# Moving the low parts of the first expert's weights from VectorE to GpSimd

## The chip, the cores and the metric

The program runs on one core of a Trainium2 chip. The metric is the device time of one execution in microseconds (us). Before the change three runs took 922.83, 923.97 and 923.83 us, median 923.83 us.

## The reference

Three layers follow each other, all in fp32: attention, a feed-forward layer and a mixture of experts.

```python
x = (out_up + out_local)            # attention, 4 x 8 heads, 576 x 64; x becomes (2304, 512)
h = x @ w_in                        # (512, 2048)
g = h * tanh(softplus(h))
x = g @ w_out                       # (2048, 512)
logits = x @ w_gate + modality_bias[modality_id]      # 8 experts
e_idx = argmax(logits, axis=1)
out[token] = gate_w * (relu(x @ w1[e]) @ w2[e])       # w1[e] (512, 1024), w2[e] (1024, 512)
```

## The kernel before

Products in fp32 are made of three products each: every operand is split into a high part, rounded to the matmul's format, and a low part, the rest (raw minus high). ScalarE copies the high part (a cast), another engine subtracts to get the low part, and TensorE adds up high x high, high x low and low x high.

The feed-forward layer works on 6 blocks of 384 tokens (NTB = 6), and in each block on 16 slabs of 128 hidden columns (NF = 16). For slab j TensorE makes `ffn_in(j)` (12 matmuls, L1308, L1309, L1314) into one of four PSUM banks and then `ffn_out(j - 2)` (9 matmuls, L1333 to L1335). `ffn_out(c)` waits for the low part of g, `g_lo` (L943). Between the two stands the nonlinearity, an exchange of ScalarE and VectorE over one slab: ScalarE Exp (L729), VectorE L992 and L994 (tensor_scalar, scalar_tensor_tensor, both from SBUF to SBUF), ScalarE Ln and Exp (L738, L740), VectorE L999 and L1002. VectorE makes the low part of the slab before, g (L943), behind L994; ScalarE makes its high part (L752) behind the Exp of L729. The order on each engine is written out by hand and repeats for each j.

In the first block GpSimd also makes the low parts of four late weight slabs (`split_lo`, L542), each released by two ScalarE casts (L679). For the rest of the layer GpSimd makes the low parts of x (L562), once in a block.

In the last block ScalarE does one more thing in the iterations j = 8 to 15, ahead of L729: `expert_hi` (L716), two casts of 128x512 of a slab of the first expert (NES = 8 slabs of w1 and w2). SyncE loads the slabs into a ring of four buffers (`wsraw`); the load of slab c waits until the low part of slab c - 4 is made (`ws_lo` >= c - 3). VectorE makes the low parts, `first_expert_lo(c)`, at the end of iteration c + 9, and the last one behind the block. Its second-last call stands between L1002 of j = 15 and the last L943, on which the last `ffn_out` waits.

Behind the block come the gate logits of the last 384 tokens, and the routing: TensorE (L1408 to L1423), VectorE (L1050 to L1163) and GpSimd (L582 to L598, which starts with a wait on `rt_gate`). The rank matmuls (L1408) and L1104 also wait for all eight low parts, `ws_lo` >= 8. Then the experts' tiles follow.

Of the kernel before, what the change touches and what calls it, by code (L numbers as in the profile page):

```python
# [14 lines left out]
ALU = mybir.AluOpType  # L15
ACT = mybir.ActivationFunctionType
AXX = mybir.AxisListType.X
F32 = mybir.dt.float32
# [10 lines left out]
def wait(eng, sem, n):  # L29

    if not (isinstance(n, int) and n <= 0):
        eng.wait_ge(sem, n)


def build(nc, q, k, v, w_in, w_out, modality, w_gate, mbias, w1, w2, out):
    B, H, S, D = q.shape
    DM, FF = w_in.shape
# [21 lines left out]
    TB, NTB = 384, N // 384  # L59
# [14 lines left out]
    with ctx:  # L74
# [3 lines left out]
        def sem(name):  # L78
            return ctx.enter_context(nc.semaphore(name))
# [61 lines left out]
        NRAW = 4  # L141
        NES = NC2
        before1 = [0]

        def alloc1(name, shape, dt=F32):
            n = 1
            for d_ in shape[1:]:
                n *= d_
            before1[0] += (n * (2 if dt == BF16 else 4) + 31) // 32 * 32
            return alloc(ctx, name, shape, dt)  # L150

        wsraw = alloc1("wsraw", [P, NRAW, 2 * DM])
# [47 lines left out]
        def bank(b, n=BANK):  # L200
            return ps[:, b * BANK:b * BANK + n]
# [9 lines left out]
        def e_part(slab, which, part):  # L211

            return WD[:, ds(slab * SLAB + (which * 2 + part) * DM, DM)]
# [112 lines left out]
        ws_hi = sem("ws_hi")  # L326
        ws_lo = sem("ws_lo")
# [33 lines left out]
        LATE = NF - NES  # L361
# [134 lines left out]
        def _(pool):  # L496
# [82 lines left out]
                               pattern=[[1, P]], channel_multiplier=-1).then_inc(rt_consts, 1)  # L579


            pool.wait_ge(rt_gate, 1)  # L582
            rest = r18[:, 3, :]
            for n in range(3):
# [247 lines left out]
        def _(dve):  # L832
# [17 lines left out]
            for m, dst in enumerate((bia, lg)):  # L850
                last = dve.tensor_tensor(
                    dst[:, :].rearrange("p (i e) -> p i e", e=E),
                    mb_sb[:, m * E:(m + 1) * E].unsqueeze(1).to_broadcast([P, NTOK, E]),
                    modf[:, m, :].unsqueeze(2).to_broadcast([P, NTOK, E]), ALU.mult)
# [85 lines left out]
            def g_part_lo(c, par):  # L940
                dve.wait_ge(g_hi, c + 1)
                wait(dve, mm2, c - 1)
                dve.tensor_tensor(gl[:, par, :], Eb[:, par, :], gh[:, par, :].bitcast(F32), ALU.subtract  # L943
                                  ).then_inc(g_lo, 1)

            def gate_copy(qn):
                dve.wait_ge(y_turned, qn + 1)
                wait(dve, logit_mm, qn)
                dve.tensor_copy(yT[:, :, :].rearrange("p a b -> p (a b)"), bank(7)).then_inc(yT_out, 1)

            def gate_out(qn):
                dve.wait_ge(logit_mm, qn + 1)
                dve.tensor_tensor(lg[:, ds(qn * E, E)], bank(7, E), bia[:, ds(qn * E, E)], ALU.add
                                  ).then_inc(logit_out, 1)

            def first_step(n):

                wait(dve, e_first, n)
                if n == 0:
                    ins = dve.tensor_reduce(first[:, 0, 0:1], lg[0:1, 0:E], AXX, ALU.max)  # L960
                elif n == 1:
                    ins = dve.tensor_tensor(first[:, 1, :], lg[0:1, 0:E], first[:, 0, 0:1].to_broadcast([1, E]),
                                            ALU.subtract)
                elif n == 2:
                    ins = dve.scalar_tensor_tensor(out=first[:, 2, :], in0=first[:, 1, :], scalar=0.0,
                                                   in1=rev[0:1, :], op0=ALU.is_ge, op1=ALU.mult)
                elif n == 3:
                    ins = dve.tensor_reduce(first[:, 0, 1:2], first[:, 2, :], AXX, ALU.max)
                else:
                    dve.tensor_scalar(first_i[:, :], first[:, 0, 1:2], -1.0, float(E), ALU.mult, ALU.add  # L970
                                      ).then_inc(first_expert, 1)
                    return
                ins.then_inc(e_first, 1)

            def first_expert_lo(c):

                dve.wait_ge(ws_hi, c + 1)
                for which in range(2):
                    last = dve.tensor_tensor(e_part(c, which, 1), wsraw[:, c % NRAW, which * DM:(which + 1) * DM],
                                             e_part(c, which, 0).bitcast(F32), ALU.subtract)  # L980
                last.then_inc(ws_lo, 1)

            def ffn_block(i, before):

                for j in range(NF):
                    c = i * NF + j
                    par = j % 2
                    Ec, Tc, Rc, hc = Eb[:, par, :], Tb[:, par, :], Rb[:, par, :], bank(j % 4, TB)
                    dve.wait_ge(e_done, c + 1)
                    wait(dve, ln_done, c - 1)  # L990
                    wait(dve, n_done, c - 1)
                    dve.tensor_scalar(Tc, Ec, ECLAMP, 2.0, ALU.min, ALU.add).then_inc(a_done, 1)  # L992
                    dve.wait_ge(a_done, c + 1)
                    dve.scalar_tensor_tensor(out=Tc, in0=Ec, scalar=ECLAMP, in1=Tc, op0=ALU.min, op1=ALU.mult  # L994
                                             ).then_inc(t_done, 1)
                    if j >= 1 or before is not None:
                        g_part_lo(c - 1, 1 - par)
                    dve.wait_ge(t_done, c + 1)
                    dve.tensor_tensor(Ec, Tc, hc, ALU.mult).then_inc(n_done, 1)  # L999
                    dve.wait_ge(n_done, c + 1)  # L1000
                    dve.wait_ge(r_done, c + 1)
                    dve.tensor_tensor(Ec, Ec, Rc, ALU.mult).then_inc(g_done, 1)  # L1002
                    if isinstance(i, int) and i == NTB - 1 and j < 5:
                        first_step(j)
                    if isinstance(i, int) and i == NTB - 1 and j > LATE:
                        first_expert_lo(j - LATE - 1)
                    if before is not None:
                        if j in (2, 4, 6):
                            gate_copy(before * NS + j // 2 - 1)
                        if j in (3, 5, 7):  # L1010
                            gate_out(before * NS + j // 2 - 1)

            ffn_block(0, None)
            with dve.Fori(1, NTB - 1) as i:
                ffn_block(i, i - 1)
            ffn_block(NTB - 1, NTB - 2)
            g_part_lo(NTB * NF - 1, (NF - 1) % 2)
            first_expert_lo(NES - 1)

            step = [0]  # L1020

# [52 lines left out]
            dve.sem_inc(rt_gate, 1)  # L1074

            CNT, TILES, USED, _, START, RANK, END, TMP = range(8)
            dve.wait_ge(rt_rank, 1)
            link(dve.tensor_reduce(e8[:, CNT, :], bank(1, NTOK * E).rearrange("p (i e) -> p e i", e=E), AXX, ALU.add))
# [441 lines left out]
```

## Time and profile before

| what | value |
|---|---|
| median of 3 runs | 923.83 us |
| the profiled execution's own time | 922.83 us |
| its span, first to last instruction | 921.1 us |
| TensorE (PE) busy | 852.1 us, 93% |
| VectorE (DVE) busy | 506.0 us, 55% |
| ScalarE (ACT) busy | 429.7 us, 47% |
| GpSimd (POOL) busy | 210.7 us, 23% |
| mean granted TensorE clock | 0.972 |

The profile is of one execution. Its rows name the engine, the line of the kernel and the tiles; times are microseconds from the span's start, durations in the grouped rows are nanoseconds. An engine's instructions are printed with their full length, though the next one can start before the last has written its end. GpSimd stands idle for nearly all of the last block, which lasts from about 568 to 644 us.

### The profile page before, as it was taken

What the parts mean: (1) busy time and instruction counts of PE and PEld (TensorE: products, weight loads), DVE (VectorE), ACT (ScalarE), POOL (GpSimd) and SP (SyncE); (2) the same over time, 40 slices, a digit from 0 to 9 for tenths busy, and PEclk for the clock granted to TensorE, in tenths of its full rate; (3) what the DMA queues carried; (4) which work ended last, traced back from release to release, by engine and by line L of the source; (5) the groups of instructions that cost most, each with busy time, mean ns of one, the idle gap of its engine ahead of it and who ended that gap; (6) DMA issues with size and microseconds to landing.
All of it is one profiled execution on the core that took longest, in us unless ns stands there. A gap on an engine that the chain in (4) does not pass through costs nothing.

```text
span 921.1 us, 16050 instructions
## 1 busy us (share of the span) xinstructions
PE 852.1 (93%) x4845; PEld 727.6 (79%) x4846; DVE 506.0 (55%) x1039; ACT 429.7 (47%) x1186; POOL 210.7 (23%) x202
## 2 busy tenths in 40 slices
PE   5787888888999999999999999999699999999994
PEld 3566666667998998998988998998578888888883
DVE  6999999963665565555555555568762111111110
ACT  3777767773555345445445445466053222222221
POOL 2566767643121001001001002000311111111110
PEclk9999999987999999999999999999899999999998
DMA  5555555320100000000000000212060111111110
GB/s 114 145 150 141 146 141 144 95 56 25 47 23 35 1 1 35 0 0 10 24 0 0 34 0 0 90 60 69 35 229 35 46 46 37 42 46 46 38 42 13
DMA packets 88197, 51.57 MB, mean 56 GB/s; under 512 B 64480, under 2 KB 77280, under 8 KB 88160
## 3 DMA queue, kind: packets, MB, share of 16 engines
q1 hardware_dynamic: 85040, 41.16, 16.0%
q0 software_dynamic: 3120, 9.96, 3.2%
q8 instruction: 17, 0.28, 0.1%
q14 instruction: 20, 0.16, 0.1%
HBM read 41.67 MB, written 9.70 MB: 56 GB/s over the span
## 4 chain that ended last, share of the span: by engine, by line
PE 77%; DVE 13%; issue 4%; ACT 2%; SPq 1%; POOL 1%; DVEq 1%; DMA 0%; ACTq 0%; POOLq 0%
PE ps L1443 8%; PE ps L1445 8%; PE ps L1444 8%; PE ps L1333 7%; PE ps L1334 7%; PE ps L1335 7%; PE ps L1309 7%; PE ps L1308 7%; PE ps L1314 7%; DVE ssum L895 3%; DVE smax L885 3%; DVE kdz L870 2%; PE ps L1234 2%; PE ps L1466 2%; PE ps L1350 1%
## 5 line engine op out<-in xcount | busy, mean ns | idle before, releaser
L729 ACT ACTIVATE Eb<-ps 128x384 f32<-128x384 f32 x96 | 47.2, 492 | 145.9 <-PE ps L1314 145.7
L992 DVE TENSOR_SCALAR Tb<-Eb 128x384 f32<-128x384 f32 x96 | 35.4, 369 | 131.1 <-ACT Eb L729 131.1
L659 ACT ACTIVATE prob<-ps,nmax 96x111 f32<-96x111 f32 (+1 forms) x256 | 87.8, 356 | 26.5 <-DVE nmax L889 26.3
L1309 PE MATMUL ps<-xh,WA 128*128 128x384 f32 x288 | 98.5, 342 | 0.0
L1308 PE MATMUL ps<-xh,WA 128*128 128x384 f32 x288 | 97.8, 340 | 0.0
L562 POOL TENSOR_TENSOR xl<-xT,xh 128x384 fp32r<-128x384 f32 x24 | 26.8, 1145 | 280.3 <-ACT xh L701 280.3
L1333 PE MATMUL ps<-WA,gh 128*128 128x512 f32 x216 | 86.8, 402 | 0.2 <-DVE gl L943 0.2
L1335 PE MATMUL ps<-WA,gl 128*128 128x512 f32 x216 | 85.4, 395 | 0.0
L1334 PE MATMUL ps<-WA,gh 128*128 128x512 f32 x216 | 85.2, 394 | 0.0
L738 ACT ACTIVATE Rb<-Tb 128x384 f32<-128x384 f32 x96 | 50.4, 525 | 60.8 <-DVE Tb L994 60.8
L1174 DVE TENSOR_TENSOR hTl<-ps,hTh 128x1024 fp32r<-128x1024 f32 x19 | 23.3, 1224 | 97.6 <-ACT hTh L792 97.6
L1002 DVE TENSOR_TENSOR Eb<-Eb,Rb 128x384 f32<-128x384 f32 x96 | 53.7, 560 | 32.9 <-ACT Rb L740 32.9
L535 POOL TENSOR_TENSOR prob<-prob,srec 96x666 f32<-96x666 f32 (+1 forms) x48 | 61.6, 1289 | 23.8 <-DVE srec L898 23.8
L1443 PE MATMUL ps<-WD,hTh 128*128 x152 | 61.4, 404 | 2.5 <-DVE hTl L1174 2.5
L1314 PE MATMUL ps<-xl,WA 128*128 128x384 f32 x288 | 62.4, 337 | 0.0
L1443 PE MATMUL ps<-WD,xTh 128*128 (+1 forms) x152 | 61.5, 405 | 0.9 <-DVE xTl L1169 0.9
L1169 DVE TENSOR_TENSOR xTl<-ps,xTh 128x512 fp32r<-128x512 f32 x20 | 13.8, 691 | 88.0 <-ACT xTh L782 88.0
L1445 PE MATMUL ps<-WD,xTl 128*128 (+1 forms) x152 | 59.6, 392 | 0.0
L1444 PE MATMUL ps<-WD,hTh 128*128 x152 | 59.5, 391 | 0.0
L1445 PE MATMUL ps<-WD,hTl 128*128 x152 | 59.4, 391 | 0.0
L994 DVE SCALAR_TENSOR_TENSOR Tb<-Eb,Tb 128x384 f32<-128x384 f32 x96 | 57.5, 599 | 3.3
L1444 PE MATMUL ps<-WD,xTh 128*128 (+1 forms) x152 | 59.3, 390 | 0.0
(218 smaller groups left out, 2009.1 us busy)
## 6 DMA issues: line engine op xcount, KB each, us to landing
wsraw<-in_moe_w_dram SPq DMA_DIRECT2D x32, 256.0 KB, 3.3
vwin<-in_v_dram SPq DMA_DIRECT2D x32, 166.5 KB
qraw<-in_q_dram SPq DMA_DIRECT2D x32, 144.0 KB, 3.0
kraw<-in_k_dram SPq DMA_DIRECT2D x32, 144.0 KB, 3.1
vdraw<-in_v_dram SPq DMA_DIRECT2D x32, 144.0 KB
y_rows<-yrow SPq DMA_DIRECT2D x6, 768.0 KB, 3.6
wraw<-in_moe_w_in_dram SPq DMA_DIRECT2D x12, 256.0 KB, 5.6
wraw<-in_moe_w_out_dram SPq DMA_DIRECT2D x12, 256.0 KB, 3.4
```

The costliest lines, as they stand in the source:

```text
L535: pool.tensor_tensor(pr, pr, srec[0:np_, a.s6, 0:n].unsqueeze(2).to_broadcast([np_, n, w]), ALU.mult).then_inc(normed, 1)
L659: last = act.activation(prob[0:np_, a.s6, n * w:(n + 1) * w], ps[0:np_, o:o + w], ACT.Exp, scale=sc, bias=nmax[0:np_, a.s6, n:n + 1], accu ...
L994: dve.scalar_tensor_tensor(out=Tc, in0=Ec, scalar=ECLAMP, in1=Tc, op0=ALU.min, op1=ALU.mult).then_inc(t_done, 1)
L1308: pe.matmul(dst, hi, xh[:, kk, :], start=(kk == 0), stop=False)
L1309: pe.matmul(dst, lo, xh[:, kk, :], start=False, stop=False)
L1314: last = pe.matmul(dst, hi, xl[:, kk, :], start=False, stop=(kk == NK - 1))
L1333: pe.matmul(bank(4 + s), hi, w_part(j, 1, 0), start=(j == 0), stop=False)
L1334: pe.matmul(bank(4 + s), hi, w_part(j, 1, 1), start=False, stop=False)
L1335: last = pe.matmul(bank(4 + s), lo, w_part(j, 1, 0), start=False, stop=(j == NF - 1))
L1443: pe.matmul(dst, th[:, a:b], weights(off, slab, which, 0), start=(n == 0), stop=False)
L1444: pe.matmul(dst, th[:, a:b], weights(off, slab, which, 1), start=False, stop=False)
L1445: last = pe.matmul(dst, tl[:, a:b], weights(off, slab, which, 0), start=False, stop=(n == len(slabs) - 1))
```

## The change

The call sites of `first_expert_lo` in VectorE's last block are taken out, and GpSimd gets a loop over the eight slabs with the same two subtractions of 128x512 each, the same wait (`ws_hi`) and the same signal (`ws_lo`). The loop stands in GpSimd's program behind the constants (L578) and ahead of the wait on `rt_gate`.

```diff
+            for c in range(NES):
+                pool.wait_ge(ws_hi, c + 1)
+                for which in range(2):
+                    last = pool.tensor_tensor(e_part(c, which, 1), wsraw[:, c % NRAW, which * DM:(which + 1) * DM],
+                                              e_part(c, which, 0).bitcast(F32), ALU.subtract)
+                last.then_inc(ws_lo, 1)
...
-            def first_expert_lo(c):
-                dve.wait_ge(ws_hi, c + 1)
-                for which in range(2):
-                    last = dve.tensor_tensor(e_part(c, which, 1), wsraw[:, c % NRAW, which * DM:(which + 1) * DM],
-                                             e_part(c, which, 0).bitcast(F32), ALU.subtract)
-                last.then_inc(ws_lo, 1)
...
-                    if isinstance(i, int) and i == NTB - 1 and j > LATE:
-                        first_expert_lo(j - LATE - 1)
...
             g_part_lo(NTB * NF - 1, (NF - 1) % 2)
-            first_expert_lo(NES - 1)
```

## Rows read from the trace of the kernel before

**Rows 1.** The chain of waits at the block's end: start us, length us, engine, tile, line.

```profile
636.47 0.71 PE ps L1314 x4
637.20 0.50 ACT Eb L729
640.37 1.28 DVE WD L979 x2
641.65 0.48 DVE gl L943
642.18 0.50 PE ps L1333
```

**Rows 2.** Timeline of the last block, iterations 8 to 11 (start, length, idle before).

```profile
605.31 1.13 ACT L716 CAST WD<-wsraw 128x512 fp32r<-128x512 f32 x2
608.41 0.36 DVE L992 TENSOR_SCALAR Tb<-Eb 128x384 f32<-128x384 f32 x1 [2.27 <-ACT Eb L729]
609.40 0.53 ACT L738 ACTIVATE Rb<-Tb 128x384 f32<-128x384 f32 x1 [0.62 <-DVE Tb L994]
...
613.59 0.53 ACT L738 ACTIVATE Rb<-Tb 128x384 f32<-128x384 f32 x1 [0.62 <-DVE Tb L994]
...
614.58 1.13 ACT L716 CAST WD<-wsraw 128x512 fp32r<-128x512 f32 x2
616.26 0.49 ACT L729 ACTIVATE Eb<-ps 128x384 f32<-128x384 f32 x1 [0.56 <-PE ps L1314]
```

**Rows 3.** The subtractions by line: duration ns min/median/max, VectorE now, GpSimd in block 0.

```profile
L979 DVE TENSOR_TENSOR WD<-wsraw,WD x16: 683/684/685, 615.3 to 642.6; 128x512 fp32r<-128x512 f32 x16
L542 POOL TENSOR_TENSOR WB<-yrow,WB x8: 1294/1352/1412, 228.5 to 267.1; 128x512 fp32r<-128x512 f32 x8
```

**Rows 4.** Timeline around two late slabs of the first block.

```profile
229.20 0.86 DVE L992 TENSOR_SCALAR Tb<-Eb 128x384 f32<-128x384 f32 x1 [1.10 <-ACT Eb L729]
230.09 1.53 DVE L994 SCALAR_TENSOR_TENSOR Tb<-Eb,Tb 128x384 f32<-128x384 f32 x1
...
239.55 1.13 ACT L679 CAST WB<-yrow 128x512 fp32r<-128x512 f32 x2
240.76 2.66 POOL L542 TENSOR_TENSOR WB<-yrow,WB 128x512 fp32r<-128x512 f32 x2 [9.55 <-ACT WB L679]
241.76 0.51 DVE L992 TENSOR_SCALAR Tb<-Eb 128x384 f32<-128x384 f32 x1 [1.46 <-ACT Eb L729]
242.30 1.53 DVE L994 SCALAR_TENSOR_TENSOR Tb<-Eb,Tb 128x384 f32<-128x384 f32 x1
243.87 0.53 ACT L738 ACTIVATE Rb<-Tb 128x384 f32<-128x384 f32 x1 [1.74 <-DVE Tb L994]
```

**Rows 5.** VectorE's groups by line, 228 to 268 us, then 605 to 640 us.

```profile
L994 DVE SCALAR_TENSOR_TENSOR Tb<-Eb,Tb 128x384 f32<-128x384 f32 x10 | 9.5, 947 | 0.3
L992 DVE TENSOR_SCALAR Tb<-Eb 128x384 f32<-128x384 f32 x10 | 4.5, 452 | 10.2 <-ACT Eb L729 10.2
...
L994 DVE SCALAR_TENSOR_TENSOR Tb<-Eb,Tb 128x384 f32<-128x384 f32 x8 | 4.5, 559 | 0.3
L992 DVE TENSOR_SCALAR Tb<-Eb 128x384 f32<-128x384 f32 x8 | 2.9, 360 | 5.2 <-ACT Eb L729 5.2
```

**Rows 6.** Timeline: VectorE's L943, then the `ffn_out` that needs its result.

```profile
621.85 0.55 DVE L943 TENSOR_TENSOR gl<-Eb,gh 128x384 fp32r<-128x384 f32 x1
...
624.44 0.39 PE L1333 MATMUL ps<-WA,gh 128*128 128x512 f32 x1
```

**Rows 7.** Timeline of ScalarE at the end of the last block.

```profile
638.71 0.52 ACT L738 ACTIVATE Rb<-Tb 128x384 f32<-128x384 f32 x1 [0.62 <-DVE Tb L994]
640.49 0.51 ACT L752 CAST gh<-Eb 128x384 fp32r<-128x384 f32 x1 [0.69 <-DVE Eb L1002]
```

**Rows 8.** Stretches: us, busy PE, PEld, DVE, ACT, POOL (instructions), PEclk, DMA, GB/s.

```profile
649.00:651.00 2.00, 0.75 (x7) 0.66 (x6) 1.12 (x5) 0.32 (x1) 0.00 (x0) 1.00 0.00 0
651.00:653.00 2.00, 1.14 (x17) 1.17 (x18) 1.36 (x5) 0.00 (x0) 0.20 (x1) 0.69 0.03 8
658.00:662.00 4.00, 0.64 (x18) 0.53 (x18) 3.82 (x2) 0.00 (x0) 4.00 (x3) 1.00 0.00 0
662.00:668.00 6.00, 4.14 (x25) 3.56 (x26) 5.21 (x20) 0.00 (x0) 2.99 (x3) 0.50 0.00 0
```

## The prediction

> **What bounds the kernel now.** I read the chain of waits first, because it says which engine a microsecond must be taken from. Through the last block it runs over TensorE's matmuls alone, until the block's last iteration; there it leaves TensorE, goes through ScalarE's Exp, the nonlinearity, VectorE's subtraction of a weight slab (L979) and the last low part of g, and returns to TensorE at 642.18 [rows 1]. So of the 16 instructions that the change takes off VectorE, two stand on the path that ends last. Then I read the timelines of the last block: one iteration is 609.40 to 613.59 on ScalarE, 4.19 us, which is TensorE's pace, and ScalarE has 0.56 us to spare in it [rows 2]. TensorE takes the low part of g 2.04 us after it is made (621.85 + 0.55 = 622.40, used at 624.44) [rows 6]. These two reserves decide what a delay costs. Last I looked for a place where GpSimd already does what it is to do, beside the same VectorE work: block 0's four late slabs [rows 3, 4, 5].
>
> **What is removed.** Per slab 2 x 684 ns on VectorE, 1.28 us as a pair [rows 1, 3]. Fourteen instructions (slabs 0 to 5 and slab 7) lie beside TensorE's work or behind the last L943 ahead of VectorE's wait for TensorE, and their removal is worth nothing. The pair at 640.37 is on the path. With it gone, the last L943 waits for its high part: L752 starts at 640.49 and takes 0.51 [rows 7], so L943 can start at about 641.05 instead of 641.57 (TensorE starts 0.61 us after that start: 642.18). Gain 0.52 us.
>
> **What is added: GpSimd's own time.** In block 0 the pair of subtractions takes 2.66 us (1352 ns median of one) [rows 3, 4], against a period of 4.19 us or more. GpSimd keeps up, the last slab would be ready long before the routing asks for it, and the loads of `wsraw` are released earlier than now. GpSimd's next wait (`rt_gate`) is queued behind the loop, and that comes later still. Cost of all this: nothing.
>
> **What is added: VectorE is held.** The rows that matter are VectorE's in block 0. While a GpSimd pair runs, L994 takes 1.53 us, otherwise 0.56; L992 takes 0.51 or 0.86, otherwise 0.36 [rows 4, 5]. This is so at all four late slabs: 4 x 1.53 + 6 x 0.56 = 9.5 us, just the 9.5 us of the group of ten [rows 5]. GpSimd's pair ends at 240.76 + 2.66 = 243.42 and L994 at 242.30 + 1.53 = 243.83: L994 gives its result 0.4 us after GpSimd is done, whenever it was issued. ScalarE's Ln, L738, starts at 243.87, which is 3.11 us after GpSimd's start [rows 4].
>
> The Trainium skill, SBUF — State Buffer, section "Who interferes with whom", states that a VectorE instruction with two SBUF inputs contends with a GpSimd instruction that reads SBUF, that the pair of ports is held for a whole instruction, and that issue order decides who blocks. By that rule the forecast holds as long as GpSimd issues first, and the trace agrees for L994 (0.97 us longer); if VectorE issued first, GpSimd would be the one that waits (the second rival below).
>
> GpSimd's pair starts 1.21 us after ScalarE's two casts start (239.55 to 240.76) [rows 4], thus always just ahead of L729 and L992 of the same iteration. In block 0 that is one iteration in three, with rest between. Here it is eight iterations in a row, and the ring is closed: the casts of iteration j stand behind L738 and L740 of iteration j - 1. From L738 to the next casts are 0.99 us (613.59 to 614.58) [rows 2]. The ring's period is therefore 0.99 + 1.21 + 3.11 = 5.31 us, 1.12 more than TensorE's 4.19.
>
> **Step by step.** j = 8: casts at 605.31 [rows 2], GpSimd 606.52 to 609.18. L992, issued at 608.41 [rows 2], meets its second half and ends at some 609.4 instead of 608.8; L738 at 609.99, late by 0.59. j = 9: casts 610.98, GpSimd 612.19, L738 612.19 + 3.11 = 615.30 against 613.59, late by 1.71. From here 5.31 an iteration: six more give 615.30 + 31.86 = 647.16 for L738 of j = 15 against 638.71 [rows 7], late by 8.45. L729 waits for the casts now, not for TensorE: in j = 10 it starts at 617.3 instead of 616.26. Behind L738 the last iteration is as it was, less the 0.52: the last `ffn_out` starts 8.45 - 0.52 = 7.93 us later, at 650.11.
>
> Does TensorE follow? The low part of slab c is ready some 3.6 us after GpSimd's start in iteration c + 1 (3.07 for L994, 0.55 for L943). For c = 9 that is 617.50 + 3.6 = 621.1 with TensorE ready at 620.5; from c = 10 on TensorE waits 1.1 us in each iteration; for c = 14, 644.05 + 3.6 = 647.65, with TensorE free at 644.4: 3.2 us idle. The 2.04 us of reserve [rows 6] are used up by j = 11, and the loss goes through.
>
> **TensorE's clock.** When TensorE had been busy for 0.75 of 2 us, the granted clock went from 1.00 to a mean of 0.69 and when it had been busy for 0.64 of 4 us, to 0.50 in the next 6 us (2.4 to 1.2 GHz) [rows 8]. The 3.2 us of idling at 644.4 are of that kind. Behind it stand 18 matmuls, two times the 2.1 us of an `ffn_out`. At half the clock for all of them the cost is 4.2 us, with no fall nothing; the nearest row is the mean of 0.69 after the shorter idling, over 4.2 us of work: between 1 and 2 us. I take 1.2, low since part of the fall may lie ahead of the matmuls. Falls in the routing (0.69, 0.50 now [rows 8]) can shift, with both signs, by up to about 1.5 us; I take 0.
>
> **Sum** against the profiled execution: 922.83 + 7.93 + 1.2 = 931.96 us, a loss of 9.13. That execution is the fastest of three; on their median the loss gives 923.83 + 9.13 = 932.96, and I forecast 933.0. Bounds: the ring's period is known to 0.1 us (L738 3.11 to 3.2 after GpSimd's start), seven times 0.7 us; the clock 0 to 4.2; the execution 1.0. Own range of this case 930 to 936.
>
> **The rivals.**
> - *The ring accumulates, but the clock doesn't fall* at the end: 923.83 + 7.93 = 931.8 us. For it: the idling of 3.2 us is shared out in pieces if TensorE reaches it later than I reckon. Against it: shorter idling sufficed [rows 8]. It lies inside the range.
> - *VectorE isn't held, not slower.* The place is L992 against GpSimd's first subtraction, the point that decides is which is issued first. L992 follows L729 by 0.52 us, and L729 can start some 0.2 us ahead of GpSimd once it waits for the casts; L992 would be issued about 0.3 us behind GpSimd. In block 0 it was 1.0 us at three slabs (240.76 to 241.76) [rows 4]. If GpSimd's wake-up takes longer here, it waits for L992 and then for L994, nobody waits for GpSimd, and what remains is the gain of 0.52: 923.3 us. Against it: a margin of 0.3 us eight times, and GpSimd's start after casts is 1.21 at this same shape.
> - *Held, but not accumulating.* If the hold of one iteration were absorbed as in block 0, where the next L729 was on time, only the last would count: 243.87 less 241.76 is 2.11 from L992 to L738, against 0.99 without (608.41 to 609.40): +1.12, less 0.52: 924.4 us. For it: block 0 shows no lasting delay. Against it: there two iterations without casts follow each slab, and ScalarE's reserve is 0.56 [rows 2], less than 1.12.
> - *Half of it*: GpSimd's second subtraction waits for L992, L994 slips in ahead, and the ring's period is about 4.8: seven times 0.6 less what the reserves take, about 4 us, 928 us. Nothing in block 0 shows it.
>
> **How the numbers follow.** Accumulating with a fall of the clock 0.55; without a fall 0.20; half of it 0.10; held once 0.06; not held 0.06; something in the routing or the clock that gains over 0.2% 0.03. A change under 0.2% (1.85 us) can't be told from none here. Slower: 0.55 + 0.20 + 0.10 = 0.85, and a little of the held-once case makes it 0.86; same 0.11; faster 0.03. Leaving out the not-held and the held-once cases and something at each edge gives 928 to 936 us.
>
> **What would show it.** Right: L994 in the last block at 1.5 us seven times, ScalarE's casts 5.3 us apart instead of 4.2, L729 waiting for nothing that TensorE does, TensorE idle about 1.1 us ahead of each `ffn_out` from c = 10 and about 3 us ahead of c = 14, its last `ffn_out` near 650, granted clock 0.5 somewhere in 646 to 653, GpSimd pairs of 2.66 us. Wrong: casts still 4.19 us apart (then nothing accumulates), L994 at 0.56, GpSimd pairs over 3 us (then it is GpSimd that is held), or a routing that is shorter or longer by more than 1.5 us.

## The result: 1% slower, as forecast

The changed kernel takes 933.05 us (median of 4 runs, 932.00 to 933.66), the kernel before beside it 923.33: a ratio of 1.0102, 95% interval 1.009 to 1.0115. A second comparison gave 932.12 against 924.04, ratio 1.0086 (1.007 to 1.0102). The forecast was 933.0, with a range of 928 to 936.

The profiled execution took 932.91 us, its span is 931.1 us.

Line numbers have moved on ScalarE and TensorE: the casts are now L724 (L716), the Exp L737 (L729), the Ln L746 (L738), the last low part of g L951 (L943), `ffn_out` L1330 to L1332 (L1333 to L1335). The timeline of the last block, over one turn from Ln to Ln (start, length, idle before and its releaser):

```profile
619.32 0.52 ACT L746 ACTIVATE Rb<-Tb 128x384 f32<-128x384 f32 x1 [2.40 <-DVE Tb L994]
620.30 1.13 ACT L724 CAST WD<-wsraw 128x512 fp32r<-128x512 f32 x2
621.33 0.48 ACT L737 ACTIVATE Eb<-ps 128x384 f32<-128x384 f32 x1
621.51 2.67 POOL L585 TENSOR_TENSOR WD<-wsraw,WD 128x512 fp32r<-128x512 f32 x2 [2.64 <-ACT WD L724]
621.85 1.18 DVE L992 TENSOR_SCALAR Tb<-Eb 128x384 f32<-128x384 f32 x1 [0.79 <-ACT Eb L737]
623.06 1.53 DVE L994 SCALAR_TENSOR_TENSOR Tb<-Eb,Tb 128x384 f32<-128x384 f32 x1
624.62 0.52 ACT L746 ACTIVATE Rb<-Tb 128x384 f32<-128x384 f32 x1 [2.40 <-DVE Tb L994]
```

Read it as a ring: Ln at 619.32, casts 0.98 later, GpSimd 1.21 after the casts, and the next Ln 3.11 after GpSimd's start. One turn is 5.30 us, where it was 4.19 [rows 2]. L737 has no bracket any more: it follows the casts and no longer waits for TensorE. GpSimd's pair ends at 624.18 and L994 at 624.59. VectorE's two instructions grouped by line, 605 to 645 us (busy, mean ns of one), answer to [rows 5]:

```profile
L994 DVE SCALAR_TENSOR_TENSOR Tb<-Eb,Tb 128x384 f32<-128x384 f32 x8 | 11.2, 1402 | 0.3
L992 DVE TENSOR_SCALAR Tb<-Eb 128x384 f32<-128x384 f32 x8 | 8.9, 1112 | 8.0 <-ACT Eb L737 8.0
```

The waits in 603 to 655 us (total, times, longest) show that it reaches TensorE: it stood still six times for the low part of g.

```profile
ACT Rb L746 <- DVE Tb L994: 18.3, 9, 2.4
PE ps L1330 <- DVE gl L951: 6.9, 6, 2.9
```

And the end of the block, in the timeline of ScalarE (the Ln of j = 7, of j = 8 and of j = 15) and of TensorE (the second-last `ffn_out`, whose first and last matmul are shown, then the last one's first):

```profile
603.14 0.53 ACT L746 ACTIVATE Rb<-Tb 128x384 f32<-128x384 f32 x1 [0.62 <-DVE Tb L994]
608.72 0.52 ACT L746 ACTIVATE Rb<-Tb 128x384 f32<-128x384 f32 x1 [1.12 <-DVE Tb L994]
...
645.77 0.52 ACT L746 ACTIVATE Rb<-Tb 128x384 f32<-128x384 f32 x1 [2.36 <-DVE Tb L994]
...
646.26 0.69 PE L1330 MATMUL ps<-WB,gh 128*128 128x512 f32 x1 [2.92 <-DVE gl L951]
...
649.74 0.44 PE L1332 MATMUL ps<-WB,gl 128*128 128x512 f32 x1
650.01 0.40 PE L1330 MATMUL ps<-WB,gh 128*128 128x512 f32 x1
```

The stretches around it (granted clock in the column behind the five engines):

```profile
645.00:648.00 3.00, 1.74 (x4) 1.40 (x5) 2.23 (x4) 1.50 (x3) 0.33 (x1) 0.73 0.00 0
648.00:650.00 2.00, 2.00 (x6) 1.57 (x5) 0.71 (x2) 0.06 (x1) 0.00 (x0) 0.55 0.00 0
```

TensorE idled for 2.92 us, the clock went to half, and nine matmuls took 3.75 us; from 650 us on the granted clock is 1.00 again.

**Where the 10.0 us of span went.** Two executions don't start the last block at the same time, so each part is measured from an event of its own trace. From the start to the Ln of j = 7: 603.14 against 604.32 (in the trace of before), -1.2. From there to the last `ffn_out`: 46.87 against 37.86 (642.18 in [rows 1]), +9.0. From there to the first product of the experts: 31.35 against 30.80, +0.6. From there to the end: 249.7 against 248.1, +1.6. The second part is the change. The other three add up to 1.0 us. They differ by as much between traces in which these parts of the program are the same (see the changed kernel again), so they are not put down to it.

In the experiments below "the block's stretch" is this second measure, from the Ln of j = 7 to the first matmul of the last `ffn_out`: 37.86 us before, 46.87 after. The ratio of a comparison is estimated from all its executions and isn't the quotient of the two medians beside it.

### The profile page after: what moved, and what is told of

Same layout as the page of the kernel before. It is cut to its first block, busy times and chain, and to the rows that moved or that the text cites. A ratio compares the mean times of both kernels' runs of the same rounds, so it can differ in the third digit from the quotient of the medians.

```text
span 931.1 us, 16050 instructions
## 1 busy us (share of the span) xinstructions
PE 860.2 (92%) x4845; PEld 733.0 (79%) x4846; DVE 506.2 (54%) x1023; ACT 429.5 (46%) x1186; POOL 232.5 (25%) x218
## 4 chain that ended last, share of the span: by engine, by line
PE 72%; DVE 16%; issue 5%; ACT 2%; DMA 2%; POOL 1%; DVEq 1%; SPq 0%; ACTq 0%; POOLq 0%
PE ps L1440 8%; PE ps L1442 8%; PE ps L1441 8%; PE ps L1330 7%; PE ps L1331 7%; PE ps L1332 7%; PE ps L1306 6%; PE ps L1305 6%; PE ps L1311 6%; DVE ssum L903 3%; DVE smax L893 3%; DVE kdz L878 2%; DMA vwin<-in_v_dram 2%; PE ps L1463 2%; PE ps L1347 1%
## 5 line engine op out<-in xcount | busy, mean ns | idle before, releaser
L992 DVE TENSOR_SCALAR Tb<-Eb 128x384 f32<-128x384 f32 x96 | 41.4, 431 | 133.9 <-ACT Eb L737 133.9
L737 ACT ACTIVATE Eb<-ps 128x384 f32<-128x384 f32 x96 | 47.1, 491 | 141.5 <-PE ps L1311 141.3
L1330 PE MATMUL ps<-WA,gh 128*128 128x512 f32 x216 | 87.1, 403 | 2.4 <-DVE gl L951 2.4
L1332 PE MATMUL ps<-WA,gl 128*128 128x512 f32 x216 | 85.4, 395 | 0.0
L746 ACT ACTIVATE Rb<-Tb 128x384 f32<-128x384 f32 x96 | 50.5, 526 | 73.5 <-DVE Tb L994 73.5
L1002 DVE TENSOR_TENSOR Eb<-Eb,Rb 128x384 f32<-128x384 f32 x96 | 53.7, 559 | 33.0 <-ACT Rb L748 33.0
L994 DVE SCALAR_TENSOR_TENSOR Tb<-Eb,Tb 128x384 f32<-128x384 f32 x96 | 64.3, 669 | 3.3
```

The source lines that it names most:

```text
L1330: pe.matmul(bank(4 + s), hi, w_part(j, 1, 0), start=(j == 0), stop=False)
L1332: last = pe.matmul(bank(4 + s), lo, w_part(j, 1, 0), start=False, stop=(j == NF - 1))
```

## The experiments

### Four slabs on GpSimd, four on VectorE

Against the kernel before. The first lines stand in GpSimd's program, the rest in VectorE's, which first waits for the slabs of GpSimd:

```diff
+            for c in range(4):
+                pool.wait_ge(ws_hi, c + 1)
...
             def first_expert_lo(c):
+                dve.wait_ge(ws_lo, c)
...
-                    if isinstance(i, int) and i == NTB - 1 and j > LATE:
+                    if isinstance(i, int) and i == NTB - 1 and j > LATE + 4:
                         first_expert_lo(j - LATE - 1)
```

> The kernel before, with slabs 0 to 3 of the first expert subtracted on GpSimd and 4 to 7 still on VectorE. Theory (a ring of period 5.3 us that eats reserves first): casts 5.3 us apart for iterations 9 to 11, then TensorE sets the pace again; TensorE waits 0.7 and 1.1 us ahead of two ffn_outs, no idling of 3 us and so no fall of the clock at the block's end, and the saving of 0.52 is not there, since VectorE's slab 6 stays on the path: 1.8 us slower than the kernel before, about 925.1. Rival (each slab costs the same): half of the change's loss, +4.9, 928.2. Rival (nothing accumulates, only the last iteration's hold counts): 923.3.

Measured: 925.81 us against 924.52, ratio 1.0008 (0.9997 to 1.0019). The timelines of ScalarE and TensorE (L745 is the Ln, L1341 the first matmul of an `ffn_out`; iterations 7 and 9 to 12, then the three `ffn_out`s that waited):

```profile
604.21 0.53 ACT L745 ACTIVATE Rb<-Tb 128x384 f32<-128x384 f32 x1 [0.62 <-DVE Tb L1002]
...
615.10 0.53 ACT L745 ACTIVATE Rb<-Tb 128x384 f32<-128x384 f32 x1 [2.24 <-DVE Tb L1002]
620.40 0.52 ACT L745 ACTIVATE Rb<-Tb 128x384 f32<-128x384 f32 x1 [2.40 <-DVE Tb L1002]
625.68 0.52 ACT L745 ACTIVATE Rb<-Tb 128x384 f32<-128x384 f32 x1 [2.39 <-DVE Tb L1002]
629.20 0.53 ACT L745 ACTIVATE Rb<-Tb 128x384 f32<-128x384 f32 x1 [0.61 <-DVE Tb L1002]
...
620.89 0.50 PE L1341 MATMUL ps<-WA,gh 128*128 128x512 f32 x1 [0.58 <-DVE gl L950]
626.17 0.50 PE L1341 MATMUL ps<-WA,gh 128*128 128x512 f32 x1 [0.86 <-DVE gl L950]
643.97 0.50 PE L1341 MATMUL ps<-WB,gh 128*128 128x512 f32 x1 [0.63 <-DVE gl L950]
```

The turns are 5.3 us while GpSimd works and 3.52 us behind it, when ScalarE catches up; what TensorE lost in its two waits stays lost. The block's stretch is 643.97 - 604.21 = 39.76, +1.90 us, where the theory had 1.8 and a price per slab 4.9. At the Ln of j = 11 ScalarE is 3.83 us late (625.68 - 604.21 = 21.47 us, where it was 17.64), and about half of that is taken up by reserves. Eight slabs make ScalarE 8.2 us late, up to the block's end, where the last `ffn_out` waits for this chain itself; there no reserve helps, and all of it counts, less the 0.5 us gained. So the price depends on where the slabs stand as well as on how many there are. The turn of 3.52 us, with neither a hold nor a subtraction of VectorE's own in it, is the shortest in these traces: the ring's reserve against TensorE's 4.19 is 0.67 us.

### GpSimd starts only behind L994

Against the changed kernel:

```diff
                 pool.wait_ge(ws_hi, c + 1)
+                pool.wait_ge(t_done, (NTB - 1) * NF + LATE + c + 1)
```

> The changed kernel, where GpSimd's pair for slab c also waits until VectorE's L994 of the same iteration is done. Theory (the loss is L992 and L994 being held, and nothing else): L992 0.36 and L994 0.56 in all iterations, casts 4.19 us apart, 922.8. Rival (any VectorE instruction with two SBUF inputs is held, so L1002 takes the place of L994): L1002 longer by up to 0.5 us, which costs the reserve of 0.56 a part and the last iteration 0.5: 923.3 to 924. Rival (the loss comes from something else of GpSimd's work, its number or its place): 933.

Measured: 925.12 us against 924.52, ratio 1.0002 (0.9991 to 1.0013). The same number of GpSimd instructions, at the same place in its program, and the loss is gone. The timeline of one iteration, then the last low part of g and the last `ffn_out` (L993, L995, L952, L1003 are L992, L994, L943, L1002 of before):

```profile
621.62 0.36 DVE L993 TENSOR_SCALAR Tb<-Eb 128x384 f32<-128x384 f32 x1 [1.20 <-ACT Eb L738]
622.02 0.56 DVE L995 SCALAR_TENSOR_TENSOR Tb<-Eb,Tb 128x384 f32<-128x384 f32 x1
622.50 0.55 DVE L952 TENSOR_TENSOR gl<-Eb,gh 128x384 fp32r<-128x384 f32 x1
622.72 3.04 POOL L586 TENSOR_TENSOR WD<-wsraw,WD 128x512 fp32r<-128x512 f32 x2 [1.15 <-DVE Tb L995]
622.96 0.55 DVE L1000 TENSOR_TENSOR Eb<-Tb,ps 128x384 f32<-128x384 f32 x1
623.80 0.81 DVE L1003 TENSOR_TENSOR Eb<-Eb,Rb 128x384 f32<-128x384 f32 x1 [0.29 <-ACT Rb L749]
...
641.94 0.98 DVE L952 TENSOR_TENSOR gl<-Eb,gh 128x384 fp32r<-128x384 f32 x1 [0.58 <-ACT gh L761]
642.97 0.50 PE L1331 MATMUL ps<-WB,gh 128*128 128x512 f32 x1 [0.76 <-DVE gl L952]
```

L952 starts before GpSimd, and now it is GpSimd's pair that takes longer, 3.04 instead of 2.66 us. L1000, which reads one operand from PSUM, is not touched. L1003 and the last L952, with both operands in SBUF, run into GpSimd's subtractions and take 0.25 and 0.43 us more. That is the first rival of the expectation: the hold moves to what has two SBUF operands. The Trainium skill, SBUF — State Buffer, section "Who interferes with whom", states that a VectorE instruction with two SBUF inputs contends with a GpSimd instruction that reads SBUF, that one with at most one SBUF input, outside the two-port modes, does not, and that issue order decides who blocks. The trace agrees: L1003 with 0.25 us more, L1000 with 0.55 us as before, and GpSimd's pair with 3.04 us where L952 came first. The block's stretch is 642.97 - 604.97 = 38.00 us (the Ln of j = 7 at 604.97), +0.1: the 0.52 us of the pair that left the path are eaten by the two holds of the last iteration (0.25 + 0.43 - 0.52 = 0.16).

### GpSimd writes and doesn't read

Against the changed kernel; this kernel leaves out the low parts of the first expert's weights:

```diff
-                for which in range(2):
-                    last = pool.tensor_tensor(e_part(c, which, 1), ..., ALU.subtract)
-                last.then_inc(ws_lo, 1)
+                pool.memset(e_part(c, 0, 1).bitcast(F32), 0.0)
+                pool.memset(wsraw[:, c % NRAW, :], 0.0)
+                pool.memset(e_part(c, 1, 1).bitcast(F32), 0.0).then_inc(ws_lo, 1)
```

> The changed kernel, where GpSimd's two subtractions per slab are replaced by three memsets that read nothing (512, 1024 and 512 elements a partition: the two low parts and the used slab buffer); the first expert's weights so lose their low parts. Theory (L994 is held because its second SBUF input and GpSimd's inputs share a read port): L994 stays at 0.56 while the memsets run; L992 may be held, by one memset at most; the ring's period is under 4.19 us and nothing accumulates: 922.8. Rival (any GpSimd instruction holds VectorE's L994 until it is done): L994 over 1 us, casts more than 4.5 us apart, 926 or more.

Measured: 925.35 us against 925.57, ratio 0.9999 (0.9989 to 1.0008). Timeline of GpSimd and VectorE in iteration 11 (L991 and L993 are L992 and L994 of before):

```profile
620.76 0.53 POOL L584 MEMSET WD<- 128x512 f32 x1 [2.33 <-ACT WD L723]
621.23 0.95 POOL L585 MEMSET wsraw<- 128x1024 f32 x1
621.29 1.10 DVE L991 TENSOR_SCALAR Tb<-Eb 128x384 f32<-128x384 f32 x1 [0.95 <-ACT Eb L736]
622.13 0.74 POOL L586 MEMSET WD<- 128x512 f32 x1
622.43 0.56 DVE L993 SCALAR_TENSOR_TENSOR Tb<-Eb,Tb 128x384 f32<-128x384 f32 x1
```

The scalar_tensor_tensor takes its 0.56 us with a memset beside it; the tensor_scalar is held by the write-only memset (1.10 instead of 0.36), and the memset behind it is held in turn (0.74 instead of 0.53). So the two instructions of VectorE are held for different reasons. A memset differs from a subtraction in more than its reads, though, and an instruction of GpSimd with one read was not run. I had expected a turn under 4.19 us, and that missed: it was 4.43 or 4.44 us in six of the seven turns from j = 8 on, and the block's stretch is +0.3 us. The change's turn is now accounted for: 3.52 us without holds (the first experiment), 0.81 for L992 (1.17 instead of 0.36) and 0.97 for L994 make 5.30. By these numbers either hold alone passes TensorE's 4.19 us by 0.1 to 0.3 (3.52 + 0.81 = 4.33, 3.52 + 0.97 = 4.49); it is the two together that pass it by 1.1. A turn with L994's hold alone was not measured.

### TensorE kept busy through its idling

Against the changed kernel:

```diff
+                if isinstance(i, int) and i == NTB - 1:
+                    pe.wait_ge(logit_out, (NTB - 1) * NS)
+                    for _ in range(12):
+                        pe.matmul(bank(7), w_part(NF - 1, 0, 0)[:, 0:P], w_part(NF - 1, 0, 0), start=True, stop=True)
                 ffn_out(i, NF - 2)
```

> The changed kernel with 12 matmuls of 512 columns (results unused) ahead of the wait of the second-last ffn_out, which fill TensorE's 2.9 us of idling. Theory: the granted clock stays at 1.00 through the last two ffn_outs, the second-last takes 2.1 us instead of 3.9, the last starts 1.8 us earlier against GpSimd's last pair: 931.2, give or take 1.5 for falls in the routing that move. Rival (the fall has nothing to do with the idling): 933.0.

Measured: 931.20 us against 924.52, ratio 1.0067 (1.0049 to 1.0086). Timeline of TensorE: the filling matmuls and the first matmuls of the last two `ffn_out`s.

```profile
645.97 2.89 PE L1362 MATMUL ps<-WB 128*128 128x512 f32 x12
649.07 0.50 PE L1330 MATMUL ps<-WB,gh 128*128 128x512 f32 x1 [0.20 <-DVE gl L951]
...
651.51 0.50 PE L1330 MATMUL ps<-WB,gh 128*128 128x512 f32 x1
```

The second-last `ffn_out` runs at full clock, and then TensorE waits a little for the last low part of g. The block's stretch is 651.51 - 605.88 = 45.63 us, 1.24 shorter than in the first trace of the changed kernel. By itself this looked like a confirmation, and 931.20 us was the time expected. But the next run has the same stretch without the filling matmuls, so the gain is not shown to come from them. Nor does the stretch decide the time of one execution: this profiled one took 934.09 us, the longest of its six, and 2.8 us of that lie ahead of the block (the Ln of j = 7 at 605.88, in the next run at 603.05).

### The changed kernel again

No edit.

> The changed kernel again, beside the kernel before on the same chip. Theory: from L738 of j = 7 to the last ffn_out 47.0 us as in the first trace (37.9 before), and from the first expert product to the end 249.8 us, as in all traces but that of the kernel before (248.1), so that the 1.7 us there are not the change's: +9.2, ratio 1.0100. Rival (the tail is longer by the change): before keeps 248.1 in no run and the ratio is 1.012.

Measured: 932.12 us against 924.04, ratio 1.0086 (1.007 to 1.0102). Timelines of ScalarE and TensorE, then the stretches at the same place:

```profile
603.05 0.53 ACT L746 ACTIVATE Rb<-Tb 128x384 f32<-128x384 f32 x1 [0.62 <-DVE Tb L994]
...
646.14 0.50 PE L1330 MATMUL ps<-WB,gh 128*128 128x512 f32 x1 [2.88 <-DVE gl L951]
648.58 0.50 PE L1330 MATMUL ps<-WB,gh 128*128 128x512 f32 x1
```

```profile
645.00:648.00 3.00, 1.86 (x8) 1.56 (x9) 2.13 (x5) 1.56 (x3) 0.20 (x1) 1.00 0.00 0
648.00:650.00 2.00, 1.90 (x9) 1.26 (x8) 0.68 (x2) 0.34 (x1) 0.00 (x0) 1.00 0.00 0
```

The same kernel, the same idling of 2.9 us, and no fall of the clock. The expectation of a stretch of 47.0 missed: it is 648.58 - 603.05 = 45.53 us. So the fall at this place happened in one execution and not in another, and cost 46.87 - 45.53 = 1.3 us where it did. The tail, from the experts' first product to the end, came out as expected, 929.1 - 679.29 = 249.8 us. Tails of 248.1 and 248.2 us are in the trace of before and in one experiment (GpSimd on every second slab), 249.7 to 250.0 in the eight others, two of which have all slabs on VectorE: the +1.6 of the first comparison is not the change's. The clock accounts for it. The stretches around the last matmuls, of this run (the last one ends at 919.96) and of before (911.89):

```profile
912.00:920.00 8.00, 7.38 (x24) 5.62 (x24) 0.44 (x1) 0.00 (x0) 0.00 (x0) 0.79 0.09 33
...
908.00:912.00 4.00, 3.90 (x18) 2.85 (x16) 0.00 (x0) 0.00 (x0) 0.00 (x0) 1.00 0.00 0
```

In all eight traces with the longer tail the granted clock is at half for 3.4 us among these matmuls, and in the two with the shorter one it falls only behind the last. Half the clock over 3.4 us of work is 1.7 us.

### GpSimd on every second slab

Against the kernel before. GpSimd takes slabs 0, 2 and 4 with a semaphore of its own, VectorE the others, slabs 6 and 7 behind the last low part of g:

```diff
-                wait(sp, ws_lo, c - NRAW + 1)
+                if c >= NRAW:
+                    sp.wait_ge(ws_lp if c % 2 == 0 else ws_lo, (c - NRAW) // 2 + 1)
...
+            for c in (0, 2, 4):
+                pool.wait_ge(ws_hi, c + 1)
...
+                last.then_inc(ws_lp, 1)
...
-                    if isinstance(i, int) and i == NTB - 1 and j > LATE:
+                    if isinstance(i, int) and i == NTB - 1 and j - LATE - 1 in (1, 3, 5):
...
             g_part_lo(NTB * NF - 1, (NF - 1) % 2)
+            dve.wait_ge(ws_lp, 3)
+            first_expert_lo(NES - 2)
             first_expert_lo(NES - 1)
+            dve.sem_inc(ws_lo, 3)
```

> GpSimd takes slabs 0, 2 and 4 of the first expert only (iterations 8, 10, 12), VectorE slabs 1, 3 and 5 at the ends of iterations 10, 12 and 14, and slabs 6 and 7 behind the last low part of g. Theory (a ring with a reserve that comes back): each hold makes the casts late by 1.1 us, the iteration without a hold gives 0.56 back, TensorE never waits for a low part of g before the last iteration; last ffn_out within 0.5 us of where the kernel before has it, measured from L738 of j = 7 (37.9 us), time within 0.1% of before. Rival (a price per slab, taken from the four slabs of the first experiment): 3/4 of 1.9 us, less 0.5, +0.9; rival (a price per slab from the whole change's 9.2 us for eight): +3.4.

Measured: 924.42 us against 924.04, ratio 1.0005 (0.9994 to 1.0016). Timeline (L747 is the Ln, L1003 is L994 and L988 is L979 of before; iterations 7, 12, 14 and 15, and the last `ffn_out`):

```profile
604.03 0.53 ACT L747 ACTIVATE Rb<-Tb 128x384 f32<-128x384 f32 x1 [0.62 <-DVE Tb L1003]
...
626.18 1.52 DVE L1003 SCALAR_TENSOR_TENSOR Tb<-Eb,Tb 128x384 f32<-128x384 f32 x1
...
636.77 1.29 DVE L988 TENSOR_TENSOR WD<-wsraw,WD 128x512 fp32r<-128x512 f32 x2
...
638.95 0.52 ACT L747 ACTIVATE Rb<-Tb 128x384 f32<-128x384 f32 x1 [0.95 <-DVE Tb L1003]
...
641.88 0.50 PE L1345 MATMUL ps<-WB,gh 128*128 128x512 f32 x1
```

L1003 is held twice, in iterations 10 (1.53 us) and 12, and the block's stretch is 641.88 - 604.03 = 37.85 us. From the Ln of j = 7 to that of j = 15 it is 34.92 us instead of 34.39, 0.53 late, and slab 6 behind the last low part of g gives that back (its own experiment is the next). Only 0.2 of the 0.53 is left over from the holds. The other 0.33 is VectorE's own: L1001 of j = 15, whose input is ready at some 637.64, starts at 637.97, behind the pair of slab 5. This also answers why block 0 showed no lasting delay: the hold is the same, but it has two iterations to heal.

### Slab 6 behind the last low part of g, all on VectorE

Against the kernel before:

```diff
-                    if isinstance(i, int) and i == NTB - 1 and j > LATE:
+                    if isinstance(i, int) and i == NTB - 1 and NF - 1 > j > LATE:
                         first_expert_lo(j - LATE - 1)
...
             g_part_lo(NTB * NF - 1, (NF - 1) % 2)
+            first_expert_lo(NES - 2)
             first_expert_lo(NES - 1)
```

> The kernel before with everything on VectorE, but in the last iteration slab 6's subtraction stands behind the last low part of g instead of ahead of it. Theory: this is the whole gain that the change could have had; the last ffn_out starts 0.5 us earlier after L1002, 922.8 against 923.3. Rival (the pair wasn't on the path): no shift of the last ffn_out against L1002, 923.3.

> The kernel before with slab 6's subtraction behind the last low part of g, a second time. Theory: 0.5 us faster, ratio 0.9994; from L738 of j = 15 to the last low part of g 2.3 us instead of 2.9. Rival: the 0.5 us are lost again in the routing, ratio 1.0000.

Measured: 924.24 against 924.52 us, ratio 0.9987 (0.9974 to 1.0), and the second time 923.23 against 924.04, ratio 0.9981 (0.9969 to 0.9994). Timeline of the second run's end:

```profile
638.74 0.53 ACT L738 ACTIVATE Rb<-Tb 128x384 f32<-128x384 f32 x1 [0.62 <-DVE Tb L994]
...
641.06 0.56 DVE L943 TENSOR_TENSOR gl<-Eb,gh 128x384 fp32r<-128x384 f32 x1 [0.58 <-ACT gh L752]
641.54 1.89 DVE L979 TENSOR_TENSOR WD<-wsraw,WD 128x512 fp32r<-128x512 f32 x3
...
641.68 0.51 PE L1334 MATMUL ps<-WB,gh 128*128 128x512 f32 x1
```

From the Ln of j = 15 to the last `ffn_out` 2.94 us, where it was 3.47 (638.71 to 642.18, [rows 1, 7]): 0.53 us less, where the sum had 0.52 for the pair on the path. The block's stretch is 37.33, 0.53 us less than before. The time tells less: the second interval excludes 1, the first ends at it, and both hold the 0.9994 that 0.53 us make. All that the change could have won needed no second engine, only another order on the first.

## Why the prediction was right

**What bounds, and the gain.** The pair of L979 on the path is worth 0.52 us: measured 0.53 and 0.54 with the reorder alone. The other fourteen instructions were worth nothing.

**The hold.** Forecast: L994 1.5 us in seven iterations and Ln 3.11 us behind GpSimd's start. Measured 1.50 to 1.53 seven times, and 3.11. L994 is not held beside GpSimd's memsets (0.56 us), which speaks for GpSimd's reads as the cause; that the hold follows whoever overlaps is shown by the delayed start. The words "whenever it was issued" claim more than the rows show: in all 66 held cases of the ten traces L994 starts 1.53 to 1.55 us behind GpSimd's start and ends 0.41 or 0.42 us behind its pair. L992 ahead of it is what evens that out. Issued 0.3 to 1.0 us behind GpSimd's start, it ends 1.5 us behind it. The sum doesn't suffer, since it used the 3.11 us as a whole.

**The ring.** Forecast 5.31 us a turn, measured 5.30. The stretch grew by 7.67 us where the clock stayed up, against 7.93 in the sum. The 0.26 too much are 0.09 at the entry, where j = 8 was reckoned 0.59 late and was 0.50 (603.14 to 608.72, against 604.32 to 609.40), 0.15 in the seven turns (5.29 us each) and 0.02 behind them. The reserve was reckoned at 0.56 us and is 0.67, which the sum doesn't use. That it is a ring with reserves and not a price per slab is shown by the counts: 8 slabs 7.7 us, 4 slabs 1.9, 3 slabs spread out 0.2 at the end of the exchange.

**TensorE.** Forecast idling of 0.6 us for c = 9, 1.1 us an iteration from c = 10 and 3.2 before c = 14; the trace has 0.57, turns of 5.30 against 4.19 (brackets of 0.85, since the modelled ends of matmuls overlap) and 2.92.

**The clock, right in the mean and wrong as a statement.** The sum has 1.2 us for a fall as if it came every time. It came in one of two traces, for 1.3 us, and not in the other after the same idling. A fair term was a coin's toss between 0 and 1.3, which would have given 932.4 rather than 933.0; the two medians, 933.05 and 932.12, lie around it. How often it falls over many executions stays open, since only the profiled ones show where the clock fell. Thirteen executions of the changed kernel, those of the first comparison among them, lie from 930.92 to 933.66 us, median 932.63. So the forecast had the mechanism and its size, and that the first median came within 0.1 us of 933.0 is luck: between the medians the loss was 9.72 us in the first comparison and 8.08 in the second, against 9.13 forecast.

**The rest of the program** was taken as unchanged, and is: the routing differs by 0.6 us and the tail by 1.6 between single traces, and the like differences stand between executions in which this part of the program is the same (routing 30.6 to 31.4 us, tail 248.1 to 250.0). The tail is a second place where the clock falls in some executions. The trace of before is one of the two where it didn't, and the forecast took its base from the median of three and not from this one.

The rivals: not held (GpSimd second) is refuted for the change by every L994, but it exists, as L952 against GpSimd in the delayed start shows. Held but healed is what block 0 and, but for 0.2 us, every second slab show, and what eight in a row don't. The half-way rival (L994 slipping in between GpSimd's two subtractions) is refuted by L994's 1.50 to 1.53 us.

## What to carry to other kernels

An idle engine is not a free one: before work is moved to GpSimd, look in the trace for VectorE's instructions in the moment when GpSimd runs something like it, and compare their lengths there with those elsewhere. Then ask what triggers the moved work: here ScalarE's casts start GpSimd just ahead of the one pair of VectorE instructions that ScalarE waits for next, so the collision comes every time and the delay feeds back into its own trigger. A delay below the ring's reserve (0.67 us a turn here) heals and a larger one accumulates, so the price isn't proportional to the count; and if one instruction is on the path, first try to move it behind its neighbour on the same engine.

## What the runs showed of the hardware beyond the expectation

- The hold works both ways, by order of issue: GpSimd's pair of subtractions took 2.66 us when it came first and 3.04 when VectorE's L943 came first.
- A held scalar_tensor_tensor is done 0.41 or 0.42 us after GpSimd's pair, in all 66 cases; it was always issued within GpSimd's second subtraction, about 0.3 us after that one's start.
- VectorE's tensor_scalar (0.36 us) is held even by a memset of GpSimd that reads nothing (up to 1.20 us), scalar_tensor_tensor is not.
- The same 2.9 us of idling of TensorE was followed by half the clock in one execution (0.55 from 648 to 650 us) and by full clock in another of the same kernel.
- At the program's end the clock fell to half among the last matmuls in eight of ten traces and not in the other two, whose tails (248.1 and 248.2 us) are shorter by 1.5 us or more.
